# Value products into the score banks, 128-row inputs, and products of zeros in the opening of a fused linear-attention and two-MLP kernel

## The reference

```python
# q, k, v, f_logit: (4, 8, 768, 48)
f = 1.0 / (1.0 + np.exp(-f_logit))
for t in range(768):
    state = f[:, :, t, :, None] * state + np.einsum('bhd,bhe->bhde', k[:, :, t], v[:, :, t])
    y[:, :, t] = np.einsum('bhd,bhde->bhe', q[:, :, t], state)
x = y.transpose(0, 2, 1, 3).reshape(4, 768, 384)
xn = (x - mu) / np.sqrt(var + 1e-06) * g_ln
x = x + np.maximum(xn @ w_ch1, 0.0) @ w_ch2
h = np.maximum(x @ w_in, 0.0)
# conv_out: three taps of h along the sequence, per channel
out = (h * (1.0 / (1.0 + np.exp(-conv_out)))) @ w_out
```

## Time and profile before

| what | value |
|---|---|
| median of 3 runs | 733.29 us (732.68 to 736.22) |
| profiled execution's own time | 733.2 us |
| its span, first to last instruction | 731.5 us |
| PE busy | 698.9 us (96%) |
| DVE busy | 528.0 us (72%) |
| ACT busy | 313.6 us (43%) |
| POOL busy | 167.4 us (23%) |
| instructions | 20438 |

### The profile page before, as it was taken

The page is one execution under the profiler, slowest core; times in us unless marked ns, Lnnn a source line. Parts: engine busy times, 40 slices in busy tenths (PEclk is TensorE's granted clock), DMA queues, the critical chain, the costliest instruction groups (busy, mean ns, idle before and its releaser), DMA issues.

```text
span 731.5 us, 20438 instructions
## 1 busy us (share of the span) xinstructions
PE 698.9 (96%) x8912; PEld 653.2 (89%) x8912; DVE 528.0 (72%) x994; ACT 313.6 (43%) x604; POOL 167.4 (23%) x179
## 2 busy tenths in 40 slices
PE   3688999999999999999999999999999999999998
PEld 3467899999899999989999999999989999999997
DVE  4878899769778868848967973534387777777764
ACT  3245521522241241251152142224377676776764
POOL 8102312245144235324414514500000000000000
PEclk9759999999999999999999999999999999999999
DMA  7825601661632443243161112126110120220111
GB/s 195 184 88 154 143 3 56 172 134 56 151 116 63 75 166 89 54 132 89 56 184 57 56 57 87 56 71 200 43 38 15 61 74 1 76 74 1 38 38 37
DMA packets 22793, 62.90 MB, mean 86 GB/s; under 512 B 4240, under 2 KB 15248, under 8 KB 22704
## 3 DMA queue, kind: packets, MB, share of 16 engines
q1 hardware_dynamic: 22704, 61.60, 29.9%
HBM read 52.14 MB, written 9.45 MB: 84 GB/s over the span
## 4 chain that ended last, share of the span: by engine, by line
PE 89%; DVE 4%; issue 2%; DMA 2%; ACT 1%; SPq 1%; POOL 0%; DVEq 0%; ACTq 0%; POOLq 0%
PE bank L1095 15%; PE bank L1097 13%; PE bank L1096 13%; PE bank L1290 9%; PE bank L1292 9%; PE bank L1291 9%; PE bank L1007 8%; PE bank L1047 3%; PE bank L1043 2%; PE bank L1065 2%; PE bank L1023 1%; DMA YN<-w 1%; PE bank L952 1%; PE bank L1000 1%; PE bank L1079 1%
## 5 line engine op out<-in xcount | busy, mean ns | idle before, releaser
L688 ACT ACTIVATE HHI<-bank 128x384 fp32r<-128x384 f32 x96 | 47.2, 492 | 185.3 <-PE bank L1097 185.0
L1267 DVE SCALAR_TENSOR_TENSOR TB<-HB,CW,TB 128x440 f32<-128x440 f32 x112 | 75.8, 677 | 50.3 <-ACT TB L1230 48.3
L1095 PE MATMUL bank<-XH,W1H 128*128 128x384 f32 x288 | 101.1, 351 | 0.7 <-ACT W2L L708 0.7
L1095 PE MATMUL bank<-HHI,W2H 128*128 128x384 f32 x288 | 101.3, 352 | 0.0
L1097 PE MATMUL bank<-HHI,W2L 128*128 128x384 f32 x288 | 97.2, 338 | 0.0
L1097 PE MATMUL bank<-XH,W1L 128*128 128x384 f32 x288 | 96.9, 336 | 0.0
L1096 PE MATMUL bank<-XL,W1H 128*128 128x384 f32 x288 | 96.8, 336 | 0.0
L1096 PE MATMUL bank<-HLO,W2H 128*128 128x384 f32 x288 | 96.8, 336 | 0.0
L1007 PEld LDWEIGHTS bank<-Q,K 48*64 48x64 f32 x3840 | 65.6, 143 | 18.0 <-issue 16.9
L918 DVE SCALAR_TENSOR_TENSOR HLO<-bank,HHI 128x384 fp32r<-128x384 f32 x96 | 53.0, 554 | 37.9 <-ACT HHI L688 36.6
L1007 PE MATMUL bank<-Q,K 48*64 48x32 f32 x3840 | 70.6, 227 | 9.8 <-DVE Q L795 5.6
(11 more groups left out here) (130 smaller groups left out, 1407.9 us busy)
## 6 DMA issues: line engine op xcount, KB each, us to landing
NEAR<-near SPq DMA_DIRECT2D x21, 960.0 KB, 4.8
V<-v SPq DMA_DIRECT2D x8, 576.0 KB, 7.9
x2d<-X SPq DMA_DIRECT2D x8, 576.0 KB, 4.1
F<-f SPq DMA_DIRECT2D x14, 288.0 KB, 5.0
K<-k SPq DMA_DIRECT2D x14, 288.0 KB, 6.4
Q<-q SPq DMA_DIRECT2D x14, 288.0 KB, 7.2
XB<-x2d SPq DMA_DIRECT2D x6, 663.0 KB, 5.6
out<-OB SPq DMA_DIRECT2D x6, 660.0 KB, 4.4
```

The source lines that it names most:

```text
L688: nc.scalar.activation(HHI[:, g % RA], ub[g % 2][:, 0:T], ACT.Relu).then_inc(hh_ready, 1)
L1095: mm(dst, ah, bh, start=start, stop=False, **kw)
L1267: nc.vector.scalar_tensor_tensor(out=TB[:, g % RB], in0=HB[:, g % RB, tap:tap + TB_], scalar=CW[:, g, tap:tap + 1], in1=TB[:, g % RB], op0 ...
```

## The change

- Q, K and F come from memory with all 128 rows, zeros included: one transfer where there were two of 48 rows, and no clearing of these tiles on DVE and POOL. DVE clears `AT[0]` (it was POOL's) and a part of `HLO`. `GLN` is loaded a step later, and the first four weight stages before `near`.
- In all units but the first, `y` writes to banks 5 and 6. Its state part is four products of 48 rows and 48 columns per pair of heads instead of two of 128 rows and 96 columns, all ahead of the value part. It waits for `mask` steps instead of KTOK, and the score levels 0, 1 and 3 wait for the three `xadd`.
- 15 steps `warm` on PE in the opening, of two products of zeros each, 128x384, into bank 2.
- New tables `START`, `PERIOD` and `LOADS`.

```diff
+LEVEL_AFTER_Y = (0, 1, 3)
...
         START = placed("""
-            gates1.a baseK0.a gates1.0 baseQ0.a diag0.0 sscale0.0 pT0.a baseK0.0 even0.a self0.a odd0.a
+            even0.a gates1.a baseK0.a baseQ0.a self0.a odd0.a warm0.0 diag0.0 even0.0 pT0.a gates1.0 pQ0.a
...
         LOADS = placed("""
-            W0.0 W1.0 N0.1 F0.1 W2.0 W3.0 K0.1 V0.0 Q0.1 W4.0 W5.0 W6.0 V0.1 W7.0 W8.0 F0.2 N1.1 W9.0 V0.2
+            Q0.0 G0.0 K0.0 F0.0 W0.0 W1.0 W2.0 W3.0 N0.1 V0.0 V0.1 K0.1 W4.0 F0.1 W5.0 W6.0 Q0.1 W7.0 W8.0
...
-            for chunks, gots in ((AHEAD, (f_ahead, k_ahead, q_ahead)), (REST, (f_in, k_in[0], q_in[0]))):
-                for dst, src, got, zero in zip((F, K[0], Q[0]), (f, k, q), gots, (pad_f, pad_k, pad_q)):
-                    sp.wait_ge(zero, 1 if chunks.start == 0 else 2)
-                    for par in range(2):
-                        sp.dma_start(dst[HALF * par:HALF * par + D, chunks], src[0, 0, par, :, chunks]
-                                     ).then_inc(got, 16)
-            sp.dma_start(GLN[:], g_ln).then_inc(g_in, 16)
+            for dst, src, got in ((F, f, f_ahead), (K[0], k, k_ahead), (Q[0], q, q_ahead)):
+                sp.dma_start(dst[:, AHEAD], src[0, 0, :, AHEAD]).then_inc(got, 16)
...
-            nc.gpsimd.memset(F[:, 0], 0.0).then_inc(pad_f, 1)
-            nc.gpsimd.memset(F[:, 1:], 0.0).then_inc(pad_f, 1)
...
-            nc.gpsimd.memset(AT[0][:], 0.0).then_inc(const_ready, 1)
+            pool.sem_inc(const_ready, 1)
...
-            nc.gpsimd.memset(K[1][:], 0.0).then_inc(pad_second, 1)
-            nc.gpsimd.memset(Q[1][:], 0.0).then_inc(pad_second, 1)
...
-            nc.vector.memset(K[0][:, 0], 0.0).then_inc(pad_k, 1)
-            nc.vector.memset(Q[0][:, 0], 0.0).then_inc(pad_q, 1)
-            nc.vector.memset(K[0][:, 1:], 0.0).then_inc(pad_k, 1)
-            nc.vector.memset(Q[0][:, 1:], 0.0).then_inc(pad_q, 1)
+            nc.vector.memset(HLO[:, 0].bitcast(F32), 0.0).then_inc(still_ready, 1)
+            nc.vector.memset(AT[0][:], 0.0).then_inc(at_zero, 1)
...
-                tt(X[u.par][:, c], yb[:, 0:DM], YN[:, c], ALU.add).then_inc(x_ready, 1)
+                of = pair[0][:, :, 0:NP * D].rearrange("p par (j d) -> p j par d", d=D)
+                to, near_y = (a.rearrange("p (j par d) -> p j par d", par=2, d=D) for a in (X[u.par][:, c], YN[:, c]))
+                tt(to, of, near_y, ALU.add).then_inc(x_ready, 1)
...
+            def warm(_, i):
+
+                if i == 0:
+                    pe.wait_ge(still_ready, 1)
+                for _ in range(2):
+                    mm(bank[2][:, 0:T], HLO[:, 0, 0:P], HLO[:, 0], start=True, stop=True)
...
-                elif not u.first:
-                    pe.wait_ge(copy_done[0], u.count(COPIED, 0))
+                elif u.index == 1:
+                    pe.wait_ge(copy_done[0], COPIED)
+                if u.index > 1 and st in LEVEL_AFTER_Y:
+                    pe.wait_ge(x_ready, u.count(NC, LEVEL_AFTER_Y.index(st) + 1 - NC))
...
             def y(u, c):
...
-                if not u.first:
-                    pe.wait_ge(ktok_ready, u.count(NC, c + 1))
-                elif c:
-                    pe.wait_ge(x_ready, c)
...
+                elif not u.first and u.index < NU - 1:
+                    pe.wait_ge(mask_done[0], u.count(MASKED, MASKED + LEVEL_AFTER_Y[c]))
+                if c:
+                    pe.wait_ge(x_ready, u.count(NC, c))
...
+                for j in range(NP if not new else 0):
+                    for par in range(2):
+                        rows, cols = slice(HALF * par, HALF * par + D), slice(D * par, D * par + D)
+                        for half in (slice(0, HALF), slice(HALF, C)):
+                            mm(pair[0][half, par, D * j:D * j + D], Q[u.par][rows, c, j, half], before[rows, j, cols],
+                               start=j == 0, stop=True, skip_group_check=True)
...
-                if not u.first:
-                    pe.wait_ge(x_ready, u.count(NC, c + 1))
-                elif c:
-                    pe.wait_ge(ktok_ready, c + 1)
+                pe.wait_ge(ktok_ready, u.count(NC, c + 1))
+                if u.first and c:
                     pe.wait_ge(st_ready, c)
...
+        rows = np.zeros((B, UB, 2, HALF, NC, NP, C), a.dtype)
+        rows[:, :, :, :D] = a
```

More of the change, by code:

```diff
@@ L322, in phase_a @@
         PERIOD = steps("""
[L323 to L330, removed]
+            hlo0 near0 up0 gates0 up1 sscale0 hhi0 xacc0 nsum0 hlo1 st0 hlo2 baseK0 ktr0 baseQ0 pT0 xadd0
+            pQ0 y0 sscale1 xacc1 norm0 xacc2 hlo3 kv0 hhi1 hlo4 up2 mask0 nsum1 mask1 ktok0 gates1 down0
+            hlo5 st1 pK1 neary0 up3 down1 pT1 xn0 hlo6 pQ1 up4 down2 ktr1 hhi2 score0 hhi3 xadd1 norm1 xl0
+            hlo7 pK2 up5 mask2 near1 pT2 up6 hhi4 ktok1 hhi5 pow0 mask3 down3 kv1 y1 pQ2 nsum2 down4 up7
+            xnt0 mask4 score1 up8 hhi6 down5 hhi7 up9 neary1 xh0 score2 near2 hhi8 hhi9 mask5 down6 down7
+            ktr2 hlo8 ktok2 hlo9 pow1 sscale2 pK3 xadd2 y2 copy3 kv2 pT3 pQ3 up10 st2 score3 down8 hhi10 xn1
+            pK4 up11 hhi11 pT4 xnt1 score4 xh1 norm2 pQ4 hlo10 xn2 down9 pK5 copy4 xh2 pT5 hlo11 xl1 pQ5 xl2
+            down10 copy5 xnt2 pK6 xout0 xout1 score5 pT6 xout2 neary2 pQ6 pow2 down11
             """)
@@ L363, in phase_a @@
[L363 to L371, removed]
-            wlo14.0 gates1.2 xacc2.0 xl0.0 score3.1 up2.0 up3.0 mask3.1 score4.1 near1.1 xn2.0 down0.0
@@ L378, in phase_a @@
-            pK1.2 ktok1.1 hhi5.0 hhi6.0 up7.0 st0.1 hhi7.0 pT1.2 nsum1.1 pQ1.2 up8.0 down6.0 mask0.2
-            score2.2 near2.1 hlo5.0 up9.0 mask1.2 sscale1.1 hhi8.0 up10.0 hhi9.0 down7.0 hlo6.0 xadd1.1
-            pK2.2 xnt0.1 norm0.1 pT2.2 hhi10.0 down8.0 mask2.2 pQ2.2 hlo7.0 score3.2 xh0.1 ktr2.1 mask3.2
-            hlo8.0 pow0.1 up11.0 ktok2.1 norm1.1 st1.1 pK3.2 xn0.1 sscale2.1 pT3.2 y2.1 hhi11.0 hlo9.0
-            mask4.2 neary2.1 down9.0 pQ3.2 copy3.2 mask5.2 nsum2.1 copy4.2 xh1.1 xl0.1 kv2.1 pK4.2 pow1.1
@@ new lines, in phase_a @@
+            pK1.0 wsub3.0 mask0.0 gates0.1 score1.0 pT1.0 wsub4.0 mask1.0 pQ1.0 mask2.a warm3.0 pK2.a
+            warm4.0 gates1.1 mask3.a pT2.a score2.a wlo2.0 score2.0 wsub5.0 pK2.0 warm5.0 mask2.0 pT2.0
+            pQ2.a pQ2.0 score3.a warm6.0 wsub6.0 mask3.0 mask4.a pK3.a mask5.a pT3.a pK3.0 score3.0 wlo3.0
+            pQ3.a pT3.0 wlo4.0 mask4.0 pQ3.0 pK4.a mask5.0 neary0.1 score4.a warm7.0 whi3.0 pT4.a wlo5.0
+            pQ4.a wsub7.0 score4.0 copy3.a baseK0.1 warm8.0 warm9.0 wsub8.0 whi4.0 score5.a pK4.0 copy3.0
@@ L1026, in y @@
             def y(u, c):
[L1027 to L1031 removed]
+                before, new = state(u, c - 1), c == 0 and u.half == 0
                 if u.first and c == 0:
```

126 lines of the change are left out of this document (75 added, 51 removed).

## The result

The changed kernel takes 727.4 us (median of 14 runs, 724.69 to 735.08) against 732.63 (14 runs, 729.59 to 738.18): a ratio of 0.9943 with a 95% interval of 0.9915 to 0.9970. It is faster by 0.6%, where 722 us, 1.5%, was forecast. Timed twice more it gave 730.34 us (ratio 0.9973, 0.9943 to 1.0002) and 727.80 us (0.9944, 0.9918 to 0.9969). Its single runs lie up to 10 us apart. The profiled one is its longest: 735.08 us, with a span of 733.3. So I read mechanisms from that profile, and sizes from medians.

A forecast was written before the change was run, and what follows sets the result against it. PE was taken to bound the period from 120 to 500 us, but not the opening; 733.2 - 3.9 - 1.1 - 4.0 - 1.4 - 1.0 = 721.8, forecast as 722 us, range 715 to 730.

The forecast's parts named there:

- Term 1: Opening: padded 128-row loads arrive at about 400 GB/s, so `self0.0` ends at 19.5 us against 23.36: -3.9 us.
- Term 2: Opening: `pK1.a` and the first half of `mask0.a` move into an earlier gap of DVE: -1.1 us.
- Term 3: From 23.4 to 56.7 us: products of zeros hold PE at 2.4 GHz, themselves costed at nothing: -4.0 us.
- Rival A: The clock falls back as before, so the zeros gain nothing: 726 to 727 us, chance 0.13.
- The stretch from 56.7 us to the first `up`: End of the opening: both engines full and few steps moved, so no change: 0.
- Term 4: `y` in the period: the new state part saves 0.08 us in each of 18 chunks with a state: -1.4 us.
- Term 5: Period: two returns from small to large products fewer in each of 5 periods: -1.0 us.
- The new waits: Period: score levels waiting for `xadd` cost nothing, `score2` being the tightest and just fitting: 0.
- rival E: Period: DVE is late at the score levels tied to `xadd`; 737 us if each is 1.0 us late, chance 0.10.
- Rival B: Between 56.7 and 97 us DVE is full, so half of the opening's 9.0 us is lost: 726 us, chance 0.15.

The follow-up runs named there:

- clear_late: The changed kernel with POOL's clearing of `AT[0]` for unit 2 moved behind `near1.1`: 725.39 us, ratio 0.9897.
- clear_late_2: The kernel of clear_late timed again, beside the changed kernel on one chip: 725.34 us.
- after_again: The changed kernel once more, unaltered, for a second profile: 730.34 us.
- pad_only: The kernel before with the 128-row loads alone and without the clearing; its own order and `y`, no zeros: 724.32 us, ratio 0.9882.
- no_warm: The changed kernel without the `warm` steps (30 products of zeros): 729.83 us, ratio 0.9965.
- clear_oldperiod: clear_late with `y`, its waits and `PERIOD` as in the kernel before: 726.26 us.
- pad_loads: pad_only with the change's `LOADS` and its first transfers; `START`, `y` and `PERIOD` as before: 723.29 us, ratio 0.9872.

## Why the prediction was wrong, point by point

**Term 1 (-3.9) was right in kind and failed in the place.** The rate came as taken from the earlier trace rows: 358 GB/s from 2.5 to 12.5 us, 418 from 12.5 to 16. What failed is "there at about 4.5 us". That took 2.3 us to landing from before, and here chunk 0 of Q needs 4.6. Two lines of the trace's list of transfers (KB each, us to landing), and SP's timeline:

```profile
F<-f SPq DMA_DIRECT2D x1, 256.0 KB, 2.7
...
Q<-q SPq DMA_DIRECT2D x1, 256.0 KB, 4.6
```

```profile
1.71 0.43 SPq L496 DMA_DIRECT2D Q<-q  x1
2.33 0.33 SPq L466 DMA_DIRECT2D Q<-q  x1
```

The second set goes out right behind it, but so it did before, behind Q at 3.19:

```profile
4.12 0.89 SPq L495 DMA_DIRECT2D F<-f  x2
```

Why chunk 0 of Q takes so long stays open. With the same queue it needs 3.2 us in clear_late, 3.5 in clear_late_2 and 5.3 in after_again. In this profile the first product starts at 6.35 us, no earlier than before (6.11; 5.01 in clear_late, 7.08 in after_again), `even0.0` at 10.11 (8.1 forecast), and `self0.0` on DVE is done at 22.37 (19.5 forecast, 23.36 before):

```profile
19.78 2.59 DVE L759 TENSOR_TENSOR AT<-bank,KTOK 64x512 f32<-64x512 f32 x4
```

That is -1.0 in this profile. Yet the loads alone gave 8 us. Of the 9.4 us between the two profiled spans of before and pad_only, 3.3 are there at the first `up`, near the forecast, and 5.6 come in the five periods (292.9 us before, 287.3): the prediction looked for nothing of the loads there. Before, PE has two pauses of 1.5 and 1.8 us inside a `score` in these periods, and a half-speed stretch of 3.4 us; pad_only has none. By the last section's reckoning that is some 5 of the 5.6.

**Term 2 (-1.1)** wasn't measured apart. The first half mask does start 1.2 us earlier (22.29 against 23.50), as far as `self0.0` moved.

**Term 3 (-4.0) is the step that failed most.** It said that the zeros would hold 2.4 GHz, and: "The zeros themselves I cost at nothing: they stand in PE's waits." In the change's profile, 14 of the 22 products that the term counted come ahead of 49.4 us, at 0.32 us and more instead of 0.17, and few waits are left for them to stand in. That is not the zeros' doing. no_warm, without them, is busy at 1.2 GHz nearly throughout, since the new order of `START` leaves PE little idle time:

```profile
23.40:56.70 33.30, 32.60 (x592) 23.30 (x593) 26.68 (x69) 14.76 (x34) 2.16 (x3) 1.00 0.24 77
```

So the zeros hold up the scores behind them: the first `y` is at 53.48 us with them and at 49.88 without, in two profiles that both reach 2.4 GHz late (49.4 and 55.8 us). In 11 profiles with the 15 filler steps of the change, the rise to 2.4 GHz that held came between 31.7 and 53.3 us, in five without them between 52.3 and 56.1. So fillers can bring it earlier, by up to 20 us, and don't always. In the median the two cancelled: no_warm lies 0.5 us below the change, where -4.0 had been forecast. Rival A (726 to 727, chance 0.13) describes that median; its time came out, partly for other reasons.

**The stretch from 56.7 us to the first `up`, put at 0,** holds the clearing beside XN: 2.5 us (727.80 against 725.34). The order of POOL's steps was in the diff, and "the steps that move are few" passed over one of 2.66 us.

**Term 4 (-1.4) came out in size, half of it by luck.** Two of the change's `y`, on PE:

```profile
187.41 0.68 PE L1051 MATMUL bank<-ST,Q 48*64 48x48 f32 x32
188.02 1.14 PE L1057 MATMUL bank<-V,AT 128*64 128x48 f32 x32
188.99 0.53 PE L1088 MATMUL bank<-V,KTOK 128*48 128x48 f32 x16
```

```profile
170.35 0.68 PE L1051 MATMUL bank<-ST,Q 48*64 48x48 f32 x32
170.96 1.14 PE L1057 MATMUL bank<-V,AT 128*64 128x48 f32 x32
172.03 0.44 PE L1118 MATMUL bank<-HHI,W2H 128*128 128x384 f32 x1
```

0.61 us for the state part, 19 ns a record (18 forecast). Over the 15 `y` of five periods 22.87 us against 23.95 in pad_only: -1.1 us, and 12 of them have a state, for which -0.08 each was forecast, -1.0. But a `y` with a state took 1.73 us in every place, and now takes 1.68 where a large tile follows and 1.58 where `kv` does. The state part gives 0.05 each, 0.6 in all; the other 0.5 comes from the five places where the new table has `kv2` behind `y2`. And the price of a record doesn't lie between those of 32 and 64 columns: of 32 columns or of 48, records of 48-row tiles start in fours, 58 ns from four to four. The floor of about 25 ns from start to start that the Trainium skill states (TensorE: Matmul & The Clock Gate, Wait — 56ns, not 53.3ns?) doesn't hold for these records either: within a four they start 7 ns apart.

**Term 5 (-1.0) had the wrong sign.** I counted returns "from small products back to `up` or `down`", with the transposes among the small ones. They are not: after a transpose of 128 by 128 the next 384-column product starts 0.03 us later. What costs is a change of tile size. Before it, a product of 384 columns is followed after 0.27 us instead of 0.17, a transpose after 0.20 instead of 0.03; after it, the last small record takes 0.14 to 0.15. Of such ways in `PERIOD` has 8 before and 10 after. The rule of the Trainium skill that I had cited as speaking against the change (TensorEngine Tiling (Array Packing), Key Properties: a change of mode drains the engine) is the one that held, and its price here is 0.30 us in and out. In five periods PE's work grew by 0.5 us although `y` lost 1.1, so the table added 1.6 where -1.0 was forecast. That is less than ten ways at 0.30: changes between two small sizes cost too, and the old table has more of them. A `score` starts 0.14 us after the last record of `kv`, at three places in each old period and at none in the new one. The sixth period I had not counted: 46.4 us by the new table, 48.0 by the old. With it, PE's work is 1.1 us less by the new table, and its idle time 1.9 us more.

**The new waits (0)** are small but there. PE's waits of the change from 120 to 480 us:

```profile
PE bank L1011 <- issue: 1.8, 4, 0.8
PE bank L1120 <- issue: 1.8, 1, 1.8
PE bank L1118 <- DVE HLO L913: 1.5, 3, 0.6
PE bank L1118 <- DVE XL L909: 0.7, 1, 0.7
```

None is a `score` that waits for X or Q, so rival E did not come. The second row and the last are of `START`, ahead of the mark. The 1.5 us are `up` or `down` behind a `score`, waiting for a low half that the new order makes late. Together terms 4 and 5 and the waits are -0.9 us by the medians of clear_late_2 and clear_oldperiod, within what can be told from nothing.

**Rival B (726)** gives the time of clear_late and clear_late_2, but its mechanism isn't shown. Their profiles reach the first `up` at 71.5 and 70.6 us, the forecast's 71, which is 8.7 and 9.6 us ahead of before. At the mark 8.2 and 6.1 of that are left, and these two executions took 720.85 and 722.22 us, near what the sum had said for the change. Their kernels' medians are 725.4 and 725.3 because their other executions are slower, and of those there is no profile. DVE is 22.49 of 23.5 us busy between 56.7 and 80.2 us in the change, so it can be what holds PE up; no run took work from it.

In sum, by medians: loads and their order -8 to -9.5; zeros about 0; the clearing +2.5; the new period and `y` -1 to +1. What the order of `START` costs beside these is left as the rest, about 3 us (clear_oldperiod 726.3 against pad_loads 723.3, on two chips), and wasn't tried step by step. It can hold both a cost of the order of steps and a clock that rises late: the profile of clear_oldperiod has 2.4 GHz only from 52.9 us, and its first `up` at 78.1.

## What to carry to other kernels

Time each part of a large change alone, first of all the plainest: the loads held more than the whole. Fillers for the clock aren't free where the clock has not risen yet, and one profile doesn't show what they do, since the same kernel got its 2.4 GHz at 34 us in one execution and at 53 in another. Count the places where PE changes its tile size, not the places where its products are small, and put steps of small tiles side by side, of the same size if you can; and when a step on POOL moves, look at what DVE runs beside it.
